# Moving the row-sum step of the GpSimd engine one pipeline slot later

## What is computed

```
scores = (q @ k.T) / sqrt(64)              # 4 batches, 8 heads, 576 x 576
kth    = 32nd largest score of the row
attn   = exp(scores - max) where scores >= kth, else 0
attn   = attn / (sum(attn) + 1e-9)
x = attn @ v                               # 2304 tokens x 512
x = elu(x @ w_in) @ w_out                  # 512 -> 2048 -> 512
e = argmax of the cosine of x with 8 expert vectors
out = gate * (relu(x @ w1[e]) @ w2[e])     # 512 -> 1024 -> 512
```

## Time and profile before

| | us |
|---|---|
| three runs | 1204.68, 1205.06, 1205.21 |
| their median | 1205.06 |
| the profiled execution | 1205.21 |
| its span in the profile | 1203.4 |
| PE busy | 1126.0 (94%) |
| DVE busy | 916.2 (76%) |
| ACT busy | 731.4 (61%) |
| POOL busy | 559.9 (47%) |

### The profile page before, as it was taken

The page is one execution under the profiler, slowest core; times in us unless marked ns, Lnnn a source line. Parts: engine busy times, 40 slices in busy tenths (PEclk is TensorE's granted clock), DMA queues, the critical chain, the costliest instruction groups (busy, mean ns, idle before and its releaser), DMA issues. The chain is left out here.

```text
span 1203.4 us, 24932 instructions
## 1 busy us (share of the span) xinstructions
PE 1126.0 (94%) x7783; PEld 884.2 (73%) x7783; DVE 916.2 (76%) x3405; ACT 731.4 (61%) x1721; POOL 559.9 (47%) x768
## 2 busy tenths in 40 slices
PE   4676799999999999999999999999999999999997
PEld 1444577787678778767877876778877888888886
DVE  5999999879988978998997899895158565536351
ACT  4666776676678667667856766774454454536341
POOL 4888755556655555565555566653000111121211
PEclk9766899999999999999999999999999999999999
DMA  8310011110001111000112000000062266235401
GB/s 268 74 44 10 7 25 26 34 40 7 7 23 32 26 41 32 7 7 22 32 26 52 23 7 7 22 9 1 19 233 78 65 240 232 101 121 203 156 30 41
DMA packets 80360, 73.06 MB, mean 61 GB/s; under 512 B 60454, under 2 KB 60454, under 8 KB 79728
## 3 DMA queue, kind: packets, MB, share of 16 engines
q1 hardware_dynamic: 74064, 56.11, 14.9%
q0 software_dynamic: 3520, 10.75, 2.7%
q10 hardware_dynamic: 2656, 4.74, 1.1%
HBM read 62.14 MB, written 10.22 MB: 60 GB/s over the span
## 5 line engine op out<-in xcount | busy, mean ns | idle before, releaser
L727 PE MATMUL mlp<-g,wout 128*128 128x320 f32 (+1 forms) x1024 | 276.9, 412 | 1.6 <-issue 1.3
L544 POOL TENSOR_TENSOR probs<-scores,probs 128x576 f32<-128x576 f32 x144 | 203.9, 1416 | 151.5 <-ACT probs L975 149.3
L1234 DVE MAX8 top<-larger_of 128x8 f32<-128x288 f32 x576 | 246.2, 448 | 1.4
L727 PEld LDWEIGHTS mlp<-g,wout 128*128 128x128 f32 x1024 | 185.6, 191 | 67.5 <-issue 26.2
L1243 DVE MATCH_REPLACE8 larger_of<-top,larger_of 128x288 f32<-128x288 f32 x432 | 189.1, 443 | 0.0
L718 PE MATMUL mlp<-x_h,win_h 128*128 128x256 f32 (+1 forms) x512 | 162.8, 318 | 12.4 <-DVE g L1350 7.0
L718 PE MATMUL mlp<-x_h,win_l 128*128 128x256 f32 (+1 forms) x512 | 151.3, 295 | 0.0
L718 PE MATMUL mlp<-x_l,win_h 128*128 128x256 f32 (+1 forms) x512 | 151.1, 295 | 0.0
L968 ACT COPY scores<-sc 128x288 f32<-128x288 f32 x288 | 103.3, 404 | 78.2 <-PE sc L662 63.2
L1234 DVE MAX8 top<-smaller_of 128x8 f32<-128x288 f32 x288 | 131.7, 457 | 0.0
L502 POOL TENSOR_TENSOR smaller_of<-scores 128x288 int32<-128x288 int32 x144 | 114.8, 797 | 34.8 <-ACT scores L968 18.5
(11 more groups left out here) (233 smaller groups left out, 2163.3 us busy)
## 6 DMA issues: line engine op xcount, KB each, us to landing
w_exp<-in_moe_w SPq DMA_DIRECT2D x16, 2048.0 KB, 13.3
raw_q<-in_q SPq DMA_DIRECT2D x64, 64.0 KB, 2.1
raw_k<-in_k SPq DMA_DIRECT2D x32, 128.0 KB, 2.3
vals<-in_v SPq DMA_DIRECT2D x32, 128.0 KB, 2.4
g<-in_moe_w_in SPq DMA_DIRECT2D x4, 1024.0 KB, 5.5
wout<-in_moe_w_out SPq DMA_DIRECT2D x1, 4096.0 KB, 14.5
x_rows<-g ACTq DMA_DIRECT2D x12, 256.0 KB, 2.0
x_rows<-g ACTq DMA_DIRECT2D x8, 192.0 KB, 2.1
```

The source lines that it names most:

```text
L544: pool.tensor_tensor(pr, scores[:, T % NSC, :], pr, ALU.subtract).then_inc(mask_done, 1)
L727: mm = pe.matmul(mlp_ps[bank_][:, 0:NB[blk]], wout[:, c, i * P:(i + 1) * P], g[:, c * NB[blk]:(c + 1) * NB[blk]], start=(c == 0), stop=(c ...
L1234: ins = dve.max(ranks(T, half, 8 * r, 8 * r + 8), folds(T, half))
```

## The change

The call of `total` leaves the place after `smaller` and goes to the head of the slot, and its tile index changes from `s - 3` to `s - 4`.

```diff
             for s in range(END):
+                if 0 <= s - 4 < NT and ends_group(s - 4):
+                    total(group_of(s - 4))
                 if s + 1 < NT:
                     both_halves(s + 1)
                     smaller(s + 1)
-                if 0 <= s - 3 < NT and ends_group(s - 3):
-                    total(group_of(s - 3))
                 if 0 <= s - 2 < NT:
                     mask(s - 2)
                 if 0 <= s - 4 < NT and ends_group(s - 4):
```

## The result

| | before | after |
|---|---|---|
| median of the runs, us | 1204.87 (6 runs) | 1211.58 (6 runs) |
| lowest and highest, us | 1204.33 to 1205.96 | 1210.31 to 1212.41 |
| ratio, with its 95% interval | | 1.0053 [1.0042, 1.0064] |
| the profiled execution, us | 1205.21 | 1209.67 |
| its span, us | 1203.4 | 1207.8 |

The changed kernel is slower by 0.53%, some 6.7 us between the medians. A second set of five runs of it, with a profile of its own, gave 1211.54 beside 1205.26 for the kernel before, 6.3 us, and 1.0053 [1.0039, 1.0067]. The forecast was 1210.0. The ratios compare runs taken side by side and are not the quotients of the medians; where the two differ, the ratio with its interval is the firmer.

The account below looks back on a forecast made before the run. DVE was taken to bound roughly the first 150 us, PE later. Delays passed to ACT and PE sum to 4.9 us, taking 1205.21 to 1210.1, median 1210.0; range 1205.2 to 1212.8.

Parts of the forecast that it names:

- The wait in front of `mask` gains nothing: On POOL, the 103.5 us idle before `total` become a longer wait before `mask`, which needs ACT's `drop`; gain nothing.
- The new waits on DVE: DVE's reciprocal waits for `total` in early slots, 0.70 to 1.59 us each; every late slot in full, 9.9 us.
- Its chain: On POOL, `total` now stands behind `mask`, `x_l` and `win_l`; in slot 13 it ends at 81.19, reciprocal 1.41 us late.
- The share that is passed on: Delay ACT and PE take over from DVE: 0.55, 1.0, 1.0, 1.3, 1.0 us in slots 8, 12, 16, 19, 20; sum 4.9.
- slot 21's 1.59 us "absorbed": Slot 21's late reciprocal, 1.59 us, stays on DVE alone, which has 1.86 idle us between 130 and 150 us.
- The later stretch at 0 of 0 to 2: From slot 24 on PE bounds and DVE has 88 idle us; late reciprocals cost 0, bounds 0 and 2 us.
- the likeliest case alone: The forecast of 4.9 us more, without the rivals: whole-kernel time 1208 to 1211.3 us; chance 0.52 with neighbours from 3 to 6.
- A: Rival: PE bounds, DVE falls behind by 1.6 us once, nothing is felt; 1205.1 + 0 to 1.6, about 1206; chance 0.17.
- C: Rival: ACT takes over DVE's whole delay, 6.5 us with slot 21, up to 2 later; 1211.6 to 1213.6 us; chance 0.22.
- B: Rival: in early slots PE's higher clock shortens the 20 products, added waits shrink to 0.3 us; 1202.5 us; chance 0.06.
- D: Rival: POOL is freed, `mask` starts 0.19 us earlier in at most ten early groups; 1203.2 us; chance 0.03.

## Why the prediction was right, and where its steps were off

**The wait in front of `mask` gains nothing: right.** The 103.5 us went over to L544, and the run with the late reciprocal, with POOL in the changed order, is at 1.0005.

**The new waits on DVE: right in place, a third too large in sum.** Forecast 9.9 us in eight slots, measured 7.4 in seven. Each was read off POOL's and DVE's times of the kernel before as if neither moved. In slots 15 and 19 DVE was already late from the slots before and met `total` sooner: 0.60 and none, instead of 1.16 and 1.04. By the prediction's own sum slot 23 was late too, and it left that out without a reason; these are its rows in the kernel before:

```profile
129.41 0.15 DVE L1276 RECIPROCAL rowrec<-rowsum 128x2 f32<-128x2 f32 x1
129.95 0.80 POOL L502 TENSOR_TENSOR smaller_of<-scores 128x288 int32<-128x288 int32 x1
```

That is 129.95 + 0.19 - 129.41 = 0.73 us. None was measured there, again with DVE already late.

**Its chain: incomplete.** The prediction let `total` follow `mask`, `x_l` and `win_l`, each at the pace of the kernel before. The rows above show `win_l` waiting 0.78 us for ACT's `win_h`, and the run that moved `x_l` away left the wait at 1.23. What keeps `total` late once DVE is late is ACT's delay, which is DVE's own of the slot before.

**The share that is passed on: 4.9 forecast, 5.5 measured at slot 24.** The sizes by slot are in the table; the places named, `x_high` (3.6 us of waits against 1.5) and PE's wait for `larger` of tile 20 (2.6 against 1.18), are the ones found. The delay's rise in slot 10, 0.7 us, need not be a wait at all: the two runs without a wait there, the row sums directly behind `mask` and the late reciprocal, rise by 0.9 in that slot, because their group of 20 products took 2.40 us and that of the kernel before 1.31. So it is part luck that the delay at slot 20, 4.5, came so near the forecast 4.9: smaller waits, a larger share passed on and the clock of one group offset each other.

The step that failed is the last: slot 21's 1.59 us "absorbed". It measured 1.67, and the delay rose from 4.5 to 5.5 in slot 24, by 0.9 us. PE met DVE's lateness twice on the way, in slots 23 and 24:

```profile
132.66 0.72 PE L652 MATMUL sc<-k_t,q_diag 128*128 128x288 f32 x2 [0.76 <-DVE larger_of L1230]
...
140.61 1.22 PE L662 MATMUL sc<-k_t,q_t 64*64 64x288 f32 x4 [0.71 <-DVE larger_of L1230]
```

The kernel before has neither wait. Its 1.86 idle us of DVE in the earlier trace rows came too late to help: DVE is busy 4.97 of 5 us from 130 to 135, and nearly all of the idle time lies behind that. Not all of the 0.9 need be the wait's. PE was at the lower clock level from 138.4 to 145.2 us in the changed kernel and only up to 135.6 in the kernel before, and in the second profile of the changed kernel the rise comes as 0.4 in slot 24 and 0.5 in slot 25. How it divides stays open.

**The later stretch at 0 of 0 to 2: right to half a microsecond by the traces.** 14.8 us of waits moved the delay from 5.5 to 5.9; the run with late row sums alone has +0.08% [-0.01, 0.16].

**The sum.** 4.9 were forecast between executions, the two profiles differ by 4.46, the medians by 6.7. The profiles are 1.4 us closer than the delay of 5.9 because the kernel before lost about that much to a low clock behind the pipeline in its profiled execution, and the changed kernel did not (below). The medians hold the 5.9 and 0.8 more, or 0.4 more in the second set, which no trace assigns. Both sets came out just above the prediction's span for the likeliest case alone, 1208 to 1211.3. Two ends in its text are slightly off: A's low end is 1205.1, not 1205.2, and C with half of the later stretch is 1212.6, not 1212.8.

**The rivals.** *A, PE bounds:* wrong; the Trainium skill's rule of the engine with the highest occupancy (Perfetto Trace Analysis, Identifying the Most-Contended Engine) would have pointed at PE, busy 94% of the span, and the runs with only the early and only the late row sums show DVE's wait passed on by 0.7 early and by 0.03 late; what held is its sentence that the most contended engine can change over time (same page, Optimization Strategy): here DVE early, PE later. *B, the clock makes up:* wrong in its size and in its mechanism. The prediction said that at a high clock the added waits would shrink to 0.3 us; at 0.88 the three of slots 9, 13 and 17 were 1.23. It also said that no scatter by the clock shows; with more runs there is one, below. *C, all of the delay passes:* its end at 1211.6 is where the median came out, and for slot 21 it was the better account. But it had 6.5 us of delay by then, and 5.5 were measured: DVE's last wait passed in part, not whole. *D:* no trace of it.

## What to carry to other kernels

A wait that is taken from the front of one instruction is only worth what was behind it: see first what the next instruction on that engine waits for. When a producer moves later, look at what is queued behind its reader; moving the reader down in its list, behind work that doesn't need it, undid nearly all of the loss. And look whether the delay of the reader comes back to the producer over the other engines: if it does, as here over ACT, neither the next slot nor a faster third engine makes it good, while the same waits in a stretch that another engine bounds cost next to nothing, as long as they stay within the reader's slack: 1.4 us in every group went beyond it.

## What the runs showed of the hardware

**PE's granted clock fell while PE was busy.** Behind the pipeline PE has hardly an idle time (in the kernel before it is busy 54.29 of the 56 us from 904 to 960), and in eight of the thirteen profiles its clock drops to the lower level, 1.2 GHz, once or twice for 3.4 us between 908 and 960 us. There are ten such drops, and five come behind each of two places. One is a group of products with 52 columns (L886), then 0.87 to 0.90 us in which PE waited for ACT, then wide products. In the kernel before:

```profile
940.26 2.41 PE L886 MATMUL prep_ps<-gates_at,lane_of 128*128 128x52 f32 x20
942.51 0.65 PE L815 MATMUL pv_ps<-ident,xg 128*128 128x128 f32 x4
944.03 0.47 PE L838 MATMUL sc<-w_hi,xg_h 128*128 128x512 f32 x1 [0.87 <-ACT xg_h L1127]
944.34 0.40 PE L839 MATMUL sc<-w_lo,xg_h 128*128 128x512 f32 x1
944.57 0.60 PE L838 MATMUL sc<-w_hi,xg_h 128*128 128x512 f32 x1
944.97 0.63 PE L839 MATMUL sc<-w_lo,xg_h 128*128 128x512 f32 x1
```

The same product takes 0.40 us and then 0.63. The other place has no idle time. In the second profile of the changed kernel it is twelve products of L727, 5.17 us where the kernel before had 3.48, behind a group of four columns:

```profile
911.02 2.19 PE L899 MATMUL prep_ps<-ahead_load,lane_of 128*128 128x4 f32 x17
913.53 5.17 PE L727 MATMUL mlp<-g,wout 128*128 128x320 f32 x12
```

Its windows there, with the granted clock as the third number from the end and PE busy in all of the time:

```profile
912.00:916.00 4.00, 4.00 (x22) 3.23 (x23) 3.81 (x10) 0.17 (x1) 1.15 (x1) 0.86 0.15 30
916.00:920.00 4.00, 4.00 (x16) 2.74 (x15) 3.76 (x9) 0.43 (x1) 0.00 (x0) 0.71 0.12 46
```

Each costs 1.6 to 1.7 us: 5.17 less 3.48 here, and at the other place 4.42 us from the first product of L838 to the first behind L847 in the kernel before, where the changed kernel has 2.84. The same groups, and the same 0.87 us of waiting, stand in the profiles without a drop, so they alone do not bring it about. The first profile of the changed kernel has none, the second has one, the changed kernel with the eight products two (and the highest time of its set), the kernel before one. The Trainium skill (TensorE: Matmul & The Clock Gate, Part 1) gives the lower level to an idle engine; here the trace shows no idle time in those windows, and the measurement decides, with one reserve: the ends of products are modelled in the trace, and the 17 products of four columns start 0.13 us apart (2.19 us in all), so short idle times between the narrow ones may be hidden. One or two drops would make a good part of the 3 us between executions of one kernel; only the profiled executions show whether they had one, so that is not shown for the others. It is a reason why single profiles can't settle a difference of that size.

**The early products.** Eight unused products per group raised the mean clock of 60 to 110 us from 0.66 to 0.88 and went with 1.2 to 1.3 us less than the kernel before in two sets, the second with the ten late products besides (1203.97 and 1203.91 us, 0.9989 and 0.999, the intervals ending at 1.0 and 0.9999). These are the only versions here whose interval does not reach above 1, and they gain only half of what the prediction called the least that one measurement can tell.
